# Attention with 64-query half tiles of 128 local keys, a column of ones in V, and the global queries as fifth steps of the same pipeline

## The chip, the core and the metric

The kernel runs on one core of a Trainium2 chip. The core has TensorE (PE, the matmul array, with a weight load that the profile lists as PEld), VectorE (DVE), ScalarE (ACT), GpSimd (POOL) and SyncE (SP, which here only issues DMAs). Each engine runs its own list of instructions in order; semaphores tie the lists together. The metric is the device time of one execution, in microseconds (us).

## The reference

Three layers follow each other: an attention of 512 local and 32 global positions (4 batches, 8 heads, head size 64), a routed expert layer, and a gated convolution layer. The change touches the attention alone:

```python
k_all = concat([k_g, k_l]); v_all = concat([v_g, v_l])
out_g = sm(scale * q_g @ k_all.T) @ v_all            # 32 global queries see all 544 keys
s_ll  = where(abs(i - j) <= 32, scale * q_l @ k_l.T, -1e9)
s_lg  = scale * q_l @ k_g.T                           # a local query sees 32 global keys
out_l = sm(concat([s_lg, s_ll])) @ concat([v_g, v_l]) # and local keys at most 32 away
x     = concat([out_g, out_l])                        # then expert layer, then convolution layer
# sm(s): s -= max(s); e = exp(s); e / (sum(e) + 1e-9)
```

All arithmetic here is float32.

## The kernel before

Heads are worked on in pairs: the 64 numbers of two heads lie on partitions 0 to 63 and 64 to 127. There are 16 pairs. Local queries stand in four tiles of 128 (`t`); such a tile sees 192 local keys (its own 128 and 32 on either side) and 32 global ones, 224 in all. `u` is the head within the pair.

For each pair PE does, in `period` (L717 to L724 in the listing): `scores` of the next pair (L688, eight calls of 224 columns, two heads in the two halves of the array's rows), `turn` of head 0 (probabilities transposed by an identity: L697 the first 128 keys, L699 the other 96, four calls each), `weigh` of the pair before's head 1 (L713 with the first 128 keys, L714 with the 96), `turn` of head 1, and `weigh` of head 0. In the profile a float32 matmul call is two MATMULs, and a transpose is one. The scores stand in PSUM banks 0 to 3, the transposed probabilities in banks 4 and 5 (one copy only), the results in banks 6 and 7.

DVE adds the mask and takes the negated maximum in one custom instruction for each 128x224 tile (`negated_max`, L1048), which also moves the scores to SBUF, copies bank 4 to `l_pta` (L1056), and divides a whole pair's result by the row sums (`normalize`, L1061, L1063, L1065). ACT takes the exponentials with their sums (L1395) and copies bank 5 to `l_ptb` (L1386). PE may turn the next head only when both copies are made.

After the 16 pairs the global queries follow as a phase of their own, in eight groups `k` of four heads (32 queries each, 128 rows): `g_scores` (L649, L650; 544 keys, the two pairs in the two halves of the array's columns), `g_turn` (L660, L661), `g_weigh` (L674, L676: four heads one behind the other, ten MATMULs each). Their probabilities are divided by DVE before they are turned (`g_probabilities`).

The order on each engine is the order in which the Python writes it; twelve of the sixteen periods stand in a loop. SP loads keys and queries into a ring of four pairs, and the values after; POOL issues the loads of the global phase's own keys and values (`g_k`, `g_v`), the stores of `x_rows`, and the load of `win`. Behind the attention PE transposes the rows of X for the router (`turn_tiles`, L761, then L775), and SP starts the loads of the experts' weights once the last `g_weigh` is done.

Of the kernel before, what the change touches and what calls it, by code (L numbers as in the profile page):

```python
# [37 lines left out]
WK = P + 2 * WINDOW  # L38
TK = SG + WK
VB = TK - P  # L40
# [14 lines left out]
COPY_AT = 2  # L55
PACE = 3
HIGHEST = 3.0e38
NRING = 4
PERIODS = NPAIR // NRING - 1
# [20 lines left out]
NC_CONST = C_MASK + NT * TK  # L80


def program(nc, qg, kT, v, ql, kw, va, vb, wg, w1, w2, w_in, w_out, cw, cst, out):
# [4 lines left out]
    with ctx:  # L88
# [37 lines left out]

        ends["local"] = ends["x"]

        l_q = [place("local", f"l_q{i}", [P, SL]) for i in range(NRING)]
        l_k = [place("local", f"l_k{i}", [P, NT, TK]) for i in range(NRING)]  # L130
        l_va = [place("local", f"l_va{i}", [P, NT, P]) for i in range(NRING)]
        l_vb = [place("local", f"l_vb{i}", [P, NT, P]) for i in range(NRING)]
        l_p = [[place("local", f"l_p{i}{u}", [P, NT, TK]) for u in range(2)] for i in range(2)]
        l_pta = [place("local", f"l_pta{u}", [P, NT, P]) for u in range(2)]
        l_ptb = [place("local", f"l_ptb{u}", [P, NT, P]) for u in range(2)]
        negmax = place("local", "negmax", [P, NRING, 2, NT])
        rowsum = place("local", "rowsum", [P, NRING, 2, NT])
        rowsum_e = place("local", "rowsum_e", [P, NRING, 2, NT])
        inv = place("local", "inv", [P, NRING, 2, NT])
        ends["globin"] = ends["const"]  # L140
        g_q = place("globin", "g_q", [P, NPAIR, 2 * SG])
        g_k = place("globin", "g_k", [P, NPAIR, S])
        g_v = place("globin", "g_v", [P, NPAIR, NT, P])
        g_vt = place("globin", "g_vt", [SG, NPAIR, P])
        zeros = place("globin", "zeros", [P, DM])
        ends["glob"] = ends["local"]
        g_p = [place("glob", f"g_p{i}", [P, S]) for i in range(2)]
        g_pt = place("glob", "g_pt", [P, NT + 1, P])
        g_max = place("glob", "g_max", [P, NG])
        g_negmax = place("glob", "g_negmax", [P, NG])  # L150
        g_sum = place("glob", "g_sum", [P, NG])
        g_sum_e = place("glob", "g_sum_e", [P, NG])
        g_inv = place("glob", "g_inv", [P, NG])
# [32 lines left out]
        assert ends["route"] <= ends["local"], (ends["route"], ends["local"])  # L186
# [17 lines left out]
        assert ends["globin"] <= ends["win"]  # L204
        win = place("win", "win", [P, DC, F2])
        ends["split"] = (nc.sbuf_usable_end - 2 * DC * F2 * 4) // 32 * 32
        assert ends["split"] >= ends["units"]
# [40 lines left out]
        gk_in = [sem(f"gk_in{k}") for k in range(NG)]  # L248
        gv_in = [sem(f"gv_in{k}") for k in range(NG)]
        lqk_in = [sem(f"lqk_in{i}") for i in range(NRING)]  # L250
        lv_in = [sem(f"lv_in{i}") for i in range(NRING)]
        s_ready = sem("s_ready")
        masked = sem("masked")
        max_ready = sem("max_ready")
        p_ready = sem("p_ready")
        gs_ready = sem("gs_ready")
        gmax_raw = sem("gmax_raw")
        gmax_ready = sem("gmax_ready")
        ge_done = sem("ge_done")
        gden = sem("gden")  # L260
        gp_ready = sem("gp_ready")
        gt_ready = sem("gt_ready")
        gta_copied = sem("gta_copied")
        gtb_copied = sem("gtb_copied")
        go_ready = sem("go_ready")
        t_ready = sem("t_ready")
        ta_copied = sem("ta_copied")
        tb_copied = sem("tb_copied")
        o_ready = sem("o_ready")
        den = sem("den")  # L270
        normed = sem("normed")
        xg_copied = sem("xg_copied")
# [77 lines left out]
        def of_pair(x, pair):  # L350
            return x[pair] if isinstance(pair, int) else x[bass.ds(pair, 1)].rearrange("a p s -> p (a s)")

        def load_keys(sp, pair, i):

            sp.dma_start(l_k[i][:].rearrange("p t k -> p (t k)"), of_pair(kw, pair)).then_inc(lqk_in[i], 16)

        def load_queries(sp, pair, i):
            sp.dma_start(l_q[i][:], of_pair(ql, pair)).then_inc(lqk_in[i], 16)

        def load_values(sp, pair, i):  # L360

            sp.dma_start(l_va[i][:].rearrange("p t k -> p (t k)"), of_pair(va, pair)).then_inc(lv_in[i], 16)
            sp.dma_start(l_vb[i][0:VB].rearrange("p t k -> p (t k)"), of_pair(vb, pair)).then_inc(lv_in[i], 16)

        def load_global_keys(eng, k):

            eng.dma_start(g_k[:, 2 * k:2 * k + 2], kT[2 * k:2 * k + 2].rearrange("a p s -> p a s")
                         ).then_inc(gk_in[k], 16)

        def load_global_values(eng, k):  # L370
            for a in range(2 * k, 2 * k + 2):
                eng.dma_start(g_v[:, a], v[a, 0:SL].rearrange("(c p) d -> p c d", p=P)).then_inc(gv_in[k], 16)
            eng.dma_start(g_vt[:, 2 * k:2 * k + 2], v[2 * k:2 * k + 2, SL:S].rearrange("a p d -> p a d")
                         ).then_inc(gv_in[k], 16)
# [47 lines left out]
        def _(sp):  # L422
            load_keys(sp, 0, 0)
            load_queries(sp, 0, 0)
            sp.dma_start(consts[:], cst).then_inc(const_in, 16)
            for pair in range(1, NRING):
                load_keys(sp, pair, pair)
                load_queries(sp, pair, pair)
                load_values(sp, pair - 1, pair - 1)
# [3 lines left out]
            def reload_keys(pair, i):  # L433

                sp.wait_ge(s_ready, pair + (1 - NRING + BIAS))
                load_keys(sp, pair, i)
                load_queries(sp, pair, i)

            def reload_values(pair, i):

                sp.wait_ge(o_ready, pair * 2 + (2 - 2 * NRING + BIAS))
                load_values(sp, pair, i)

            load_values(sp, NRING - 1, NRING - 1)
            reload_keys(NRING, 0)
            with sp.Fori(0, PERIODS - 1) as j:
                for i in range(NRING):
                    reload_keys(j * NRING + (NRING + 1 + i), (i + 1) % NRING)
                    reload_values(j * NRING + (NRING + i), i)
            for pair in range(NPAIR - NRING, NPAIR):  # L450
                if pair + 1 < NPAIR:
                    reload_keys(pair + 1, (pair + 1) % NRING)
                reload_values(pair, pair % NRING)
            sp.wait_ge(go_ready, NG)
# [36 lines left out]
        def _(pool):  # L491

            pool.wait_ge(pads_zero, 1)
# [3 lines left out]

            pool.wait_ge(pads_zero, 2)
            for u in range(2):
                r = slice(DH * u, DH * u + DH)  # L500
                pool.dma_start(g_q[r, :, SG * u:SG * u + SG], qg[:, r].rearrange("a p s -> p a s")).then_inc(gq_in, 16)
            def store_batch(b, pairs):
                pool.wait_ge(normed, pairs + BIAS)
# [3 lines left out]
            for k in range(NG):  # L507
                pool.wait_ge(o_ready, PACE * k + 2 + BIAS)
                load_global_keys(pool, k)
                load_global_values(pool, k)  # L510
                if k in (2, 5):
                    store_batch(k // 3, H // 2 * (k // 3 + 1))
            store_batch(2, 3 * H // 2)
            pool.wait_ge(normed, 3 * H // 2 + 2 + BIAS)
            pool.dma_start(win[:], w_in.rearrange("(c p) f -> p c f", p=P)).then_inc(win_in, 16)
            store_batch(3, NPAIR)
            pool.wait_ge(xg_copied, 1)
# [3 lines left out]
            pool.wait_ge(go_ready, NG)  # L521
# [103 lines left out]
        def _(pe):  # L625
            pe.sem_inc(s_ready, BIAS)
            pe.sem_inc(t_ready, BIAS)
            pe.sem_inc(o_ready, BIAS)
# [10 lines left out]
            def g_scores(k):  # L639
                i = k % 2  # L640
                pe.wait_ge(gk_in[k], 16)

                if k < 2:
                    pe.wait_ge(max_ready, HEADS + BIAS)
                else:
                    pe.wait_ge(ge_done, k - 1)
                for a in range(2):
                    o = slice(2 * SG * a, 2 * SG * a + 2 * SG)
                    mm(ps[o, 2 * i, :], g_q[:, 2 * k + a, :], g_k[:, 2 * k + a, 0:512], start=True, stop=True)  # L649
                    last = mm(ps[o, 2 * i + 1, 0:S - 512], g_q[:, 2 * k + a, :], g_k[:, 2 * k + a, 512:S],  # L650
                              start=True, stop=True)
                last.then_inc(gs_ready, 1)
# [10 lines left out]
            def g_weigh(k):  # L663
                b = k // 2
                if k == 0:
                    pe.wait_ge(normed, NPAIR - 1 + BIAS)
# [978 lines left out]
```

## Time and profile before

| | us |
|---|---|
| median of 3 runs | 728.49 (727.95 to 728.78) |
| the profiled execution | 729.33 |
| its span | 727.5 |
| PE busy | 670.9 (92%) |
| DVE busy | 522.7 (72%) |
| ACT busy | 366.4 (50%) |
| POOL busy | 224.1 (31%) |

The span runs from the first to the last instruction of that one execution. The chain of waits is followed back from the last instruction; a stretch that the chain gives to PE can't be shortened by any other engine. Clock 1.00 in a row means that TensorE ran at 2.4 GHz, 0.50 at 1.2 GHz.

### The profile page before, as it was taken

Reading aid. Unit: us, or ns where it says so; the run is one execution under the profiler, and the core shown is the slowest. Engines: PE = TensorE matmul, PEld = TensorE weight load, DVE = VectorE, ACT = ScalarE, POOL = GpSimd, SP = SyncE. Lnnn points to the kernel's source line nnn. Section 1 sums busy time; section 2 is a strip of 40 time slices with the busy share of each in tenths; the row PEclk is TensorE's granted clock in tenths of the full one; section 3 lists DMA queues with packets and bytes.
Section 4 is the critical chain, followed back from the end, with each engine's and each line's share of the span. In section 5 each row is a group of like instructions: output and inputs, shape, how many; then the busy total and the mean of one; then the engine's idle time right before and its main releaser. Section 6 shows DMA issues by size and latency. Waiting matters only on the chain.

```text
span 727.5 us, 12816 instructions
## 1 busy us (share of the span) xinstructions
PE 670.9 (92%) x3892; PEld 550.5 (76%) x3892; DVE 522.7 (72%) x970; ACT 366.4 (50%) x648; POOL 224.1 (31%) x189
## 2 busy tenths in 40 slices
PE   3999999899945999999999999997499999999997
PEld 2899999666434788888888888886278888888886
DVE  2667676443374989888998898894649878777672
ACT  2676776112103687777877787774242232222321
POOL 1132230002415455545554555442812011000000
PEclk9999999999965999999999999999689999999999
DMA  9989983202871010808621717400221021010102
GB/s 263 288 264 320 329 275 118 115 2 101 337 271 44 25 49 29 288 29 288 215 91 40 278 39 274 159 29 16 88 58 45 15 72 43 0 58 0 58 1 72
DMA packets 35965, 92.49 MB, mean 127 GB/s; under 512 B 3360, under 2 KB 3360, under 8 KB 35936
## 3 DMA queue, kind: packets, MB, share of 16 engines
q1 hardware_dynamic: 25024, 59.87, 24.1%
q0 software_dynamic: 7744, 26.48, 11.3%
q10 hardware_dynamic: 3168, 5.77, 2.1%
q8 instruction: 16, 0.26, 0.1%
q14 instruction: 13, 0.11, 0.0%
HBM read 76.90 MB, written 15.20 MB: 127 GB/s over the span
## 4 chain that ended last, share of the span: by engine, by line
PE 90%; DVE 4%; DMA 2%; issue 2%; POOL 1%; ACT 1%; SPq 0%; DVEq 0%; POOLq 0%; ACTq 0%
PE ps L854 20%; PE ps L856 20%; PE ps L855 20%; PE ps L714 4%; PE ps L688 4%; PE ps L713 4%; PE ps L885 3%; PE ps L674 3%; PE ps L697 2%; PE ps L775 2%; PE ps L699 2%; DMA l_q<-ql 2%; PE ps L863 1%; DVE y_g L1293 1%; PE ps L649 1%
## 5 line engine op out<-in xcount | busy, mean ns | idle before, releaser
L1444 ACT CAST w_h<-slots 128x1024 fp32r x88 | 92.0, 1049 | 47.6 <-PE ps L856 25.5
L1450 ACT CAST w_h<-slots 128x1024 fp32r x88 | 89.0, 1051 | 40.5 <-PE ps L856 27.4
L1249 DVE TENSOR_TENSOR w_l<-slots,w_h 128x1024 fp32r<-128x1024 f32 x66 | 87.6, 1375 | 12.0 <-ACT w_h L1444 8.8
L1256 DVE TENSOR_TENSOR w_l<-slots,w_h 128x1024 fp32r<-128x1024 f32 x66 | 77.8, 1230 | 16.5 <-ACT w_h L1450 16.0
L1524 ACT ACTIVATE h_buf<-ps 128x512 f32<-128x512 f32 x32 | 19.2, 601 | 123.2 <-PE ps L856 108.2
L551 POOL TENSOR_TENSOR w_l<-slots,w_h 128x1024 fp32r<-128x1024 f32 x22 | 54.6, 2483 | 73.6 <-ACT w_h L1444 73.6
L854 PE MATMUL ps<-w_h,b_hTh 128*128 128x512 f32 x176 | 71.7, 408 | 2.6 <-DVE b_hTl L1243 2.6
L854 PE MATMUL ps<-w_h,b_xTh 128*128 128x512 f32 x176 | 71.5, 406 | 1.8 <-DVE b_xTl L1236 1.6
L1048 DVE CUSTOM_DVE_ANT_0 l_p<-ps,consts 128x224 f32<-128x224 f32 x128 | 42.2, 386 | 42.9 <-PE ps L688 36.2
L558 POOL TENSOR_TENSOR w_l<-slots,w_h 128x1024 fp32r<-128x1024 f32 x22 | 57.9, 2632 | 43.0 <-ACT w_h L1450 43.0
L856 PE MATMUL ps<-w_h,b_xTl 128*128 128x512 f32 x176 | 69.9, 397 | 0.0
L855 PE MATMUL ps<-w_l,b_xTh 128*128 128x512 f32 x176 | 69.8, 396 | 0.0
L856 PE MATMUL ps<-w_h,b_hTl 128*128 128x512 f32 x176 | 69.4, 395 | 0.0
L855 PE MATMUL ps<-w_l,b_hTh 128*128 128x512 f32 x176 | 69.3, 394 | 0.0
L1395 ACT ACTIVATE l_p<-l_p,negmax 128x224 f32<-128x224 f32 x128 | 60.0, 471 | 9.7 <-DVE negmax L1048 9.3
L617 POOL COPY h_buf<-h_g 128x32 f32<-128x32 f32 x32 | 6.8, 214 | 147.3 <-DVE c_buf L1340 147.1
L854 PE MATMUL ps<-yT_h,win_h 128*128 (+1 forms) x128 | 50.6, 395 | 0.5 <-DVE yT_l L1297 0.5
L854 PE MATMUL ps<-wout_h,gl_h 128*128 128x512 f32 x128 | 51.0, 399 | 0.0
L856 PE MATMUL ps<-yT_h,win_l 128*128 (+1 forms) x128 | 50.6, 396 | 0.0
L855 PE MATMUL ps<-yT_l,win_h 128*128 (+1 forms) x128 | 50.5, 395 | 0.0
L856 PE MATMUL ps<-wout_h,gl_l 128*128 128x512 f32 x128 | 50.1, 392 | 0.0
L855 PE MATMUL ps<-wout_l,gl_h 128*128 128x512 f32 x128 | 49.9, 390 | 0.0
(225 smaller groups left out, 1503.8 us busy)
## 6 DMA issues: line engine op xcount, KB each, us to landing
slots<-w SPq DMA_DIRECT2D x16, 2048.0 KB, 11.0
l_k<-kw SPq DMA_DIRECT2D x16, 448.0 KB, 7.1
y_sorted<-b_y ACTq DMA_DIRECT2D x22, 256.0 KB, 2.9
g_k<-kT POOLq DMA_DIRECT2D x8, 544.0 KB, 5.4
l_q<-ql SPq DMA_DIRECT2D x16, 256.0 KB, 8.3
l_va<-va SPq DMA_DIRECT2D x16, 256.0 KB, 3.2
g_v<-v POOLq DMA_DIRECT2D x16, 256.0 KB, 6.6
x_rows<-X POOLq DMA_DIRECT2D x4, 1024.0 KB, 7.4
```

The source lines that it names most:

```text
L551: nc.gpsimd.tensor_tensor(w_l[:, u, :], unit_of(at, False, u), w_h[:, u, :].bitcast(F32), ALU.subtract).then_inc(w_lo_pool, 1)
L558: nc.gpsimd.tensor_tensor(w_l[:, u, :], unit_of(at, True, u), w_h[:, u, :].bitcast(F32), ALU.subtract).then_inc(w_lo_pool, 1)
L688: last = mm(ps[:, 2 * u + t // 2, at:at + TK], l_q[i][r, P * t:P * t + P], l_k[i][r, t, :], start=True, stop=True)
L854: mm(o, a_h, b_h, start=start, stop=False)
L855: mm(o, a_h, b_l, start=False, stop=False)
L856: return mm(o, a_l, b_h, start=False, stop=stop)
L1048: last = vec.tensor_tensor_reduce(out=l_p[i % 2][u][:, t, :], in0=ps[:, 2 * u + t // 2, t % 2 * TK:t % 2 * TK + TK], in1=consts[:, C_MASK ...
L1249: vec.tensor_tensor(w_l[:, u, :], unit_of(at, False, u), w_h[:, u, :].bitcast(F32), ALU.subtract).then_inc(w_lo_dve, 1)
L1256: vec.tensor_tensor(w_l[:, u, :], unit_of(at, True, u), w_h[:, u, :].bitcast(F32), ALU.subtract).then_inc(w_lo_dve, 1)
L1395: last = sca.activation(at, at, ACT.Exp, bias=negmax[:, i, u, t:t + 1], scale=-1.0, accum_out=rowsum[:, i, u, t:t + 1])
L1444: sca.copy(w_h[:, u, :], unit_of(at, False, u)).then_inc(w_hi, 1)
L1450: sca.copy(w_h[:, u, :], unit_of(at, True, u)).then_inc(w_hi, 1)
```

## The change

A tile of 128 queries is split into two halves of 64. Each half sees 128 local keys (its own 64 and 32 on either side), so that the tile is 160 columns wide (128 local, 32 global) rather than 224. The two halves go to the two halves of the array's columns, the two heads to the two halves of its rows. V gets a 65th column of ones, so that the sum of a row's exponentials comes out of the same matmul, and the divisions come after it. The values of the global keys lie in `l_vg` as a block matrix (128x260, one block for each tile), so that one call covers four tiles. Two pairs and their four heads' global queries make a group of five steps, which run in one pipeline; `g_scores` reads the keys that the local scores read. The rings get six pairs; there is no loop. PSUM banks 6 and 7 now hold one head each in turn.

```diff
-            def scores(pair, i, loads):
+            def scores(pair):
...
+                pe.wait_ge(qk_in[i], 32 * (pair // NRING + 1))
+                if pair >= 1:
+                    pe.wait_ge(max_ready, sub(pair - 1, 1) + 1)
+                    if pair % 2 == 0:
+                        pe.wait_ge(p_ready, sub_g(pair // 2 - 1) + 1)
                 for t in range(NT):
                     at = t % 2 * TK
...
+                    for u, r in enumerate(rows):
+                        mm(ps[0:HQ, 2 * u + t // 2, at:at + TK], l_q[i][r, q[0]], k[r], start=True, stop=True)
+                        mm(ps[HQ:P, 2 * u + t // 2, at:at + WK], l_q[i][r, q[1]], beside[r], start=True, stop=True)
+                    for u, r in enumerate(rows):
+                        last = mm(ps[HQ:P, 2 * u + t // 2, at + WK:at + TK], l_q[i][r, q[1]], k[r, WK:TK],
                                   start=True, stop=True)
...
+            def g_scores(g):
...
+                for a in range(2):
+                    pair = 2 * g + a
+                    k, q = l_k[pair % NRING], g_q[:, pair, :]
+                    o = slice(2 * SG * a, 2 * SG * a + 2 * SG)
+                    mm(ps[o, 0, SG:P], q, k[:, SG:P], start=True, stop=True)
+                    mm(ps[o, 0, P:SL], q, k[:, TK:NT * TK].rearrange("p (t k) -> p t k", k=TK)[:, :, 0:P],
+                       start=True, stop=True)
+                    last = mm(ps[o, 1, 0:2 * SG], q, k[:, NT * TK - SG:NT * TK + SG], start=True, stop=True)
...
+            def turn(pair, u):
...
                 for t in range(NT):
-                    last = nc.tensor.transpose(ps[0:VB, 5, P * t:P * t + P], l_p[i % 2][u][:, t, P:TK], ident)
+                    last = mm(ps[SG * t:SG * t + SG, 5, 0:P], p[:, TK * t + WK:TK * t + TK], ident,
+                              start=True, stop=True)
...
-                    mm(o, l_pta[u][:, t, :], l_va[i][:, t, d], start=True, stop=False)
-                    last = mm(o, l_ptb[u][0:VB, t, :], l_vb[i][0:VB, t, d], start=False, stop=True)
+                mm(ps[:, bank, 0:NT * VW], l_ptb[turned][:], l_vg[i][:, u].rearrange("p t d -> p (t d)"),
+                   start=True, stop=False)
+                for t in range(NT):
+                    for h in range(2):
+                        last = mm(ps[HQ * h:HQ * h + HQ, bank, VW * t:VW * t + VW],
+                                  l_pta[turned][:, t, HQ * h:HQ * h + HQ], l_va[i][:, 2 * t + h, u, :],
+                                  start=False, stop=t == NT - 1)
...
+            for g in range(NG):
+                for a in range(2):
+                    if a == 0:
+                        scores(2 * g + 1)
+                    else:
+                        g_scores(g)
+                    turn(2 * g + a, 0)
+                    if a == 1:
+                        weigh(2 * g, 1)
+                    elif g >= 1:
+                        g_weigh(g - 1)
+                    turn(2 * g + a, 1)
+                    weigh(2 * g + a, 0)
+                if g + 1 < NG:
+                    scores(2 * g + 2)
+                g_turn(g)
+                weigh(2 * g + 1, 1)
```

`g_weigh` now writes its four heads to the four quarters of the array's columns (four chunks of 128 keys, L703, and a last one of 64, L706). SP has eight DMAs for each pair rather than four: keys 352 KB, queries 256 KB, local values 520 KB, four small ones for `l_vg` (16 KB each) and one for `l_vt`. A group takes PE two `scores`, one `g_scores`, four `turn`, one `g_turn`, four `weigh` and one `g_weigh`.

PE, one pair inside the loop of the kernel before (the scores of the next pair stand at L688):

```order
52 L688 MATMUL ps<-l_k_72,l_q_68 128x224 [waits max_ready]
53 L688 MATMUL ps<-l_k_72,l_q_68 128x224 x7
54 L693 REGISTER_ALU
55 L697 MATMUL ps<-consts,l_p_81 128x128 [waits tb_copied,ta_copied,p_ready]
56 L697 MATMUL ps<-consts,l_p_81 128x128 x3
57 L699 MATMUL ps<-consts,l_p_81 96x128 x4
58 L713 MATMUL ps<-l_va_74,l_pta_86 128x64 [waits tb_copied,ta_copied]
```

PE of the kernel after, at the border of two groups (the last tile of `scores` of pair 2, `g_turn`, `weigh`, and the first tile of `scores` of pair 3):

```order
84 L629 MATMUL ps<-l_k_73,l_q_67 64x32 x2
85 L669 MATMUL ps<-consts,g_p 128x128 [waits ta_act,tb_copied,p_ready]
86 L669 MATMUL ps<-consts,g_p 128x128 x3
87 L670 MATMUL ps<-consts,g_p 64x128
88 L685 MATMUL ps<-l_vg_84,l_ptb_104 128x260 [waits normed,ta_act,tb_copied]
89 L689 MATMUL ps<-l_va_78,l_pta_102 64x65 x8
90 L626 MATMUL ps<-l_k_74,l_q_68 64x160 [waits max_ready,qk_in3]
91 L627 MATMUL ps<-l_k_74,l_q_68 64x128
```

Before, a turn and a weighing stand between two `scores` on all sides; now the `scores` of pair 3 come straight behind the weighing of pair 1's head 1, and wait for `max_ready`, the maxima of pair 2's head 1.

DVE of the kernel before, where the last maxima of a pair's head 1 are taken (L1048) and the pair before it is divided (L1061 to L1065):

```order
60 L1048 ISA l_p_82,negmax<-ps,consts 128x224
61 L1048 ISA negmax 128x1
62 L1059 ISA
63 L1061 TENSOR_SCALAR rowsum_e<-rowsum 128x8 [waits p_ready,o_ready]
64 L1062 REGISTER_ALU
65 L1063 RECIPROCAL inv<-rowsum_e 128x8 [waits den]
66 L1065 ISA [waits den]
67 L1065 TENSOR_TENSOR X<-ps,inv 128x2x4x64
68 L1055 REGISTER_ALU
69 L1056 COPY l_pta_86<-ps 128x512 [waits t_ready]
```

DVE of the kernel after, at the same border (L1028 copies the group's turned probabilities, L1035 to L1040 divide pair 1's head 1, L1012 takes the maxima of pair 2's head 1):

```order
110 L1028 COPY l_pta_102<-ps 128x512 [waits o_ready,t_ready]
111 L1035 TENSOR_SCALAR den<-ps 128x4 [waits o_ready]
112 L1037 RECIPROCAL inv<-den 128x4 [waits den_ready]
113 L1040 TENSOR_TENSOR X<-ps,inv 128x4x64 [waits inv_ready]
114 L1012 ISA l_p_98,negmax<-ps,consts 128x160 [waits t_ready,s_ready]
115 L1012 ISA negmax 128x1
116 L1012 ISA l_p_98,negmax<-ps,consts 128x160
```

Before, the maxima came ahead of the division; here the division of a head whose weighing PE has just issued stands ahead of the maxima.

## Rows read from the trace of the kernel before

**Rows 1.** The page's part 4: shares of the chain by engine

```profile
PE 90%; DVE 4%; DMA 2%; issue 2%; POOL 1%; ACT 1%; SPq 0%; DVEq 0%; POOLq 0%; ACTq 0%
```

**Rows 2.** Busy time by engine (PE, PEld, DVE, ACT, POOL), clock, DMA share, GB/s

```profile
50.00:75.00 25.00, 25.00 (x229) 23.71 (x226) 16.48 (x69) 18.25 (x67) 8.92 (x13) 1.00 0.96 306
```

**Rows 3.** The chain of waits over one period: start, us, what

```profile
59.28 1.71 PE ps L688 x16
60.99 0.59 PE ps L697 x4
61.58 0.44 PE ps L699 x4
...
63.75 0.45 PE ps L697 x4
...
66.36 1.71 PE ps L688 x16
```

**Rows 4.** The same chain at the start, in the global phase and behind the attention

```profile
2.66 12.65 DMA l_q<-ql
15.40 3.37 PE ps L688 x16
...
23.82 1.71 PE ps L688 x16
...
151.72 1.01 PE ps L649 x4
...
155.98 0.59 PE ps L660 x4
...
175.33 3.65 PE ps L761 x32
178.97 3.53 PE ps L775 x8
...
213.41 0.26 PE ps L833 x8
...
220.11 0.88 PE ps L848 x17
```

**Rows 5.** PE in time, at a change of shape: start, us, engine, line, tile, count

```profile
148.37 0.29 PE L676 MATMUL ps<-g_vt,g_pt 32*32 32x64 f32 x2
148.59 0.24 PE L674 MATMUL ps<-g_v,g_pt 128*32 128x64 f32 x1
```

**Rows 6.** DVE and PE in time, the last pair's division

```profile
132.60 0.17 DVE L1061 TENSOR_SCALAR rowsum_e<-rowsum 128x8 f32<-128x8 f32 x1 [1.00 <-PE ps L714]
132.81 0.20 DVE L1063 RECIPROCAL inv<-rowsum_e 128x8 f32<-128x8 f32 x1
133.04 0.69 DVE L1065 TENSOR_TENSOR X<-ps,inv 128x512 f32<-128x512 f32 x1
133.65 0.14 DVE L1030 TENSOR_SCALAR g_sum_e<-g_sum 128x1 f32<-128x1 f32 x1
...
134.59 0.44 PE L660 MATMUL ps<-consts,g_p 128*128 128x128 f32 x2 [2.02 <-DVE g_p L1034]
```

**Rows 7.** DVE in time, two masked maxima one behind the other

```profile
61.30 0.39 DVE L1048 CUSTOM_DVE_ANT_0 l_p<-ps,consts 128x224 f32<-128x224 f32 x1 [2.15 <-PE ps L688]
...
61.61 0.39 DVE L1048 CUSTOM_DVE_ANT_0 l_p<-ps,consts 128x224 f32<-128x224 f32 x1
```

**Rows 8.** From a turn by way of the copy to the weighing

```profile
166.31 0.27 PE L661 MATMUL ps<-consts,g_p 128*32 128x128 f32 x1
166.62 0.69 DVE L1039 COPY g_pt<-ps 128x512 f32<-128x512 f32 x1 [2.64 <-PE ps L661]
...
167.41 0.27 PE L674 MATMUL ps<-g_v,g_pt 128*32 128x64 f32 x2 [0.83 <-DVE g_pt L1039]
```

**Rows 9.** Columns as in rows 2, behind the idle stretch of rows 6

```profile
135.60:139.00 3.40, 3.40 (x24) 2.09 (x21) 2.08 (x6) 0.84 (x3) 0.00 (x0) 0.50 0.77 290
139.00:142.00 3.00, 3.00 (x34) 2.19 (x34) 0.14 (x1) 0.14 (x1) 0.00 (x0) 1.00 0.00 0
```

More of the change, by code:

```diff
@@ L135, in program @@
[L135 to L153, printed above, removed]
+        ends["ring"] = ends["const"]
@@ new lines, in program @@
+        ends["local"] = ends["x"]
+        l_p = [[place("local", f"l_p{i}{u}", [P, NT * TK]) for u in range(2)] for i in range(2)]
+        l_pta = [place("local", f"l_pta{i}", [P, NT, P]) for i in range(2)]
+        l_ptb = [place("local", f"l_ptb{i}", [P, P]) for i in range(2)]
+        g_p = place("local", "g_p", [P, GK])
+        negmax = place("local", "negmax", [P, 2, 2, NT])
+        den = place("local", "den", [P, 2, NT])
+        inv = place("local", "inv", [P, 2, NT])
+        g_max = place("local", "g_max", [P, NG])
@@ L155, in program @@
+        g_negmax = place("local", "g_negmax", [P, NG])
+        g_den = place("local", "g_den", [P, NG])
+        g_inv = place("local", "g_inv", [P, NG])
         ends["route"] = ends["x"]
@@ L348, in program @@
         storedg = sem("storedg")
[L350 to L374, printed above, removed]
+        def sub(pair, u):
+            return 5 * (pair // 2) + 2 * (pair % 2) + u
@@ L634, in _ @@
             mm = nc.tensor.matmul
[L639 to L652, printed above, removed]
@@ L715, in weigh @@
                 last.then_inc(o_ready, 1)
-            def period(p, i, loads, first=False, more=True):
-                if more:
-                    scores(p + 1, (i + 1) % NRING, loads + (1 if i + 1 == NRING else 0))
-                turn(p * 2, i, 0)
-                if not first:
-                    weigh(p + -1, (i - 1) % NRING, 1, loads - (1 if i == 0 else 0))
-                turn(p * 2 + 1, i, 1)
-                weigh(p, i, 0, loads)
-            scores(0, 0, 1)
-            pe.wait_ge(const_in, 16)
@@ L728, in _, with g_weigh @@
-            period(0, 0, 1, first=True)
-            with pe.Fori(0, PERIODS) as j:
-                for i in range(1, NRING + 1):
-                    period(j * NRING + i, i % NRING, j + (1 if i < NRING else 2))
-            for p in range(NPAIR - NRING + 1, NPAIR):
-                if p + 1 == NPAIR:
-                    pe.wait_ge(gq_in, 32)
-                    g_scores(0)
-                period(p, p % NRING, NPAIR // NRING, more=p + 1 < NPAIR)
-            for k in range(NG):
-                if k + 1 < NG:
-                    g_scores(k + 1)
-                if k == 0:
-                    weigh(NPAIR - 1, (NPAIR - 1) % NRING, 1, NPAIR // NRING)
-                else:
-                    g_weigh(k - 1)
-                g_turn(k)
+            def g_weigh(g):
+                n = sub_g(g)
+                ready_to_weigh(n)
+                bank, turned = 6 + n % 2, n % 2
+                for c in range(NT + 1):
+                    for h in range(H // 2):
+                        i, u = (2 * g + h // 2) % NRING, h % 2
+                        o = ps[SG * h:SG * h + SG, bank, 0:VW]
+                        if c < NT:
+                            mm(o, l_pta[turned][:, c, SG * h:SG * h + SG], l_va[i][:, 2 * c, u, :],
+                               start=(c == 0), stop=False)
+                        else:
+                            last = mm(o, l_ptb[turned][0:2 * SG, SG * h:SG * h + SG], l_vt[i][:, u, :],
+                                      start=False, stop=True)
+                last.then_inc(o_ready, 1)
@@ new lines, in g_normalize @@
+            def g_normalize(g):
+                n, b = sub_g(g), g // 2
+                act.wait_ge(ginv_ready, g + 1)
+                for h in range(H // 2):
+                    r, at = slice(SG * h, SG * h + SG), DH * (H // 2 * (g % 2) + h)
+                    last = sca.activation(X[SG * b:SG * b + SG, GT, at:at + DH], ps[r, 6 + n % 2, 0:DH], ACT.Copy,
+                                          scale=g_inv[r, g:g + 1])
+                last.then_inc(g_normed, 1)
+            for u in range(2):
+                exponentials(0, u)
@@ new lines, in _ @@
+            for g in range(NG):
+                for a in range(2):
+                    pair = 2 * g + a
+                    copy_turned(sub(pair, 0), P, False)
+                    if a == 0:
+                        exponentials(pair + 1, 0)
+                        if g >= 1:
+                            g_normalize(g - 1)
+                    else:
+                        g_exponentials(g)
+                    copy_turned(sub(pair, 1), P, True)
+                    if a == 0:
+                        exponentials(pair + 1, 1)
+                copy_turned(sub_g(g), 2 * SG, False)
+                if g + 1 < NG:
+                    for u in range(2):
+                        exponentials(2 * g + 2, u)
@@ new lines @@
+    values = np.ones((NPAIR, P, NX, 2, VW), np.float32)
+    for x in range(NX):
+        values[:, :, x, :, 0:DH] = padded_values[:, HQ * x:HQ * x + WK]
+    tails = np.ones((NPAIR, 2 * SG, 2, VW), np.float32)
+    tails[:, 0:SG, :, 0:DH] = global_values
+    tails[:, SG:, :, 0:DH] = local_values[:, SL - SG:]
+    global_queries = np.zeros((P, NPAIR, 2, SG), np.float32)
+    for u in range(2):
+        global_queries[DH * u:DH * u + DH, :, u] = turned(inputs["q_g"])[:, DH * u:DH * u + DH].transpose(1, 0, 2)
```

479 lines of the change are left out of this document (218 added, 261 removed).

## The prediction

> **What bounds the kernel now.** I read the chain's shares first: PE has 90% of them [rows 1]. The busy time by engine of a stretch of the local attention comes second: PE is busy for all 25.00 us, DVE for 16.5, ACT for 18.3, the 16 DMA engines for 0.96 of it [rows 2]. So PE alone sets the pace here, though the loads have little room. Third comes the chain inside one period [rows 3]: 7.08 us for a pair (66.36 - 59.28), made of scores 1.71, a first turn 0.59 + 0.44, two weighings of 1.73 (the last L699 ends at 62.02, the next L697 starts at 63.75) and a second turn of about 0.9. The global phase has a period of its own: from g_scores at 151.72 to g_turn at 155.98 [rows 4] are 4.26 us, less 1.10 for g_scores leaves 3.16 for one g_weigh; with a g_turn of 0.70 a group is 4.96 us. The whole attention runs until 175.33, where L761 begins. What lies behind it starts from semaphores that end the attention and is the same code, so that I move it as a block.
>
> **PE's prices.** A float32 matmul of 512 columns costs 3.53 / 8 = 0.441 us for each L775 [rows 4], that is 0.86 ns a column. By it the 16 matmuls of scores (224 columns, 0.193 each) would be 3.09 us one by one; they take 1.71, so the two row halves run side by side. The four L649 would be 1.76 and take 1.01: so do the two column halves. The eight L833, in four column quarters, take 0.26 us together [rows 4], 0.033 each. Rows and columns divided at once, in four quarters, no row shows. A change of shape costs: two L676 of 64 columns (0.055 each by the rate) fill 0.22 us (148.37 to 148.59) [rows 5], so about 0.10 for each change; the first turn behind scores agrees (0.59 against 0.45) [rows 3]. The Trainium skill (TensorEngine Tiling (Array Packing), Key Properties) says that a change of the tiling mode drains TensorE; it gives no time, and the trace agrees with it at those 0.10 us.
>
> **Part by part on PE.** Each call is two matmuls.
> - scores: each quarter of the array gets 320 columns a tile (2 x 160, or 2 x 128 + 2 x 32), 0.275 us, and the short ones may wait for their weights; I take 0.30. Four tiles 1.20, a weight load 0.05, a change 0.10: **1.35** against 1.71.
> - turn: four transposes 0.45 + 0.05; L662 is eight matmuls of 128 columns in four column quarters, 2 x 0.11; two changes: **0.93**, as before.
> - weigh: L685 0.11 for weights and 2 x 0.224 for 260 columns, L689 sixteen of 65 columns (0.056) in two column halves, 0.45 + 0.05, two changes: **1.25** against 1.73.
> - g_scores: 2 x 544 columns, 0.94 + 0.15: 1.08, as before. g_turn 0.70, as before.
> - g_weigh: ten matmuls of 0.057 in each quarter, three changes and weights: **0.82** against 3.16.
>
> Whole: from scores of pair 1 on, 15 x 1.35 + 8 x 1.08 + 32 x 0.93 + 8 x 0.70 + 32 x 1.25 + 8 x 0.82 = 110.8 us. Before, the same stretch is 159.9 us (175.33 - 15.40).
>
> **The wait that it adds.** At each of the seven borders of groups, PE's scores of the odd pair wait for the maxima of the even pair's head 1. DVE has the division of the weighing just issued ahead of them. So from the end of weigh: 0.2 until DVE sees it (L661, 0.11 us of columns from 166.31, answered at 166.62 [rows 8]); division 0.21 + 0.23 [rows 6] + 0.34 for 256 of 512 elements (512 are followed after 0.61; an element is (0.69 - 0.39) / 288 = 1.04 ns by [rows 6, 7]); four maxima of 160 elements at 0.245 each (0.31 at 224 [rows 7], less 64 x 1.04 ns) = 0.98, and 0.12 to be read out. PE's own drain covers 0.1. That is 0.2 + 0.78 + 1.1 - 0.1 = **2.0 us idle, 7 times, 14.0**. Behind it are queued the turns of the next group. The copy is a smaller one: L661's start to L674's is 1.10 us [rows 8]; between the end of a turn and the next one stands now a weigh of 1.25, which covers it, or a g_weigh of 0.82, which lacks 0.17: 7 x 0.17 = 1.2. DVE's load of a group is 16 maxima x 0.245, three copies x 0.61, four divisions x 0.78, g's maximum and inverse 1.2: 10.1 of some 16 us, so not the bound. ACT's exponentials get shorter and lose their sum.
>
> **The clock.** PE was idle 2.02 us at 132.6 to 134.59 [rows 6], and then stood at 0.50 for 3.4 us [rows 9]; half of that, 1.7 us, is lost. The seven new gaps are as long. Nothing else in the attention has one so long, so I can't tell how often; I take 4 of 7: **6.8 us** (0 to 11.9). At the start the first period costs 8.42 (15.40 to 23.82) where 7.08 less one weighing is 5.35 [rows 3, 4], since its scores take 3.37 at the low clock: 3.0 us, kept.
>
> **Issue.** A group has 273 matmuls (2 x 48, 4 x 12, 4 x 18, 12 + 5 + 40) in some 16 us; two pairs and a global group before had 181 (2 x 64 + 53) in 19.1. They come in bursts (48 in scores, 40 in g_weigh). Nearest row: seventeen L848 in 0.88, 0.05 each [rows 4]; the eight L833 say 0.033. At 0.05, scores behind the gap (nothing queued) would be 2.4 rather than 1.35, and g_weigh 2.0 rather than 0.82; with a little from L689 that is 2.5 a group, 20 in all. Being nearer to L833 in kind, I take 0.4 at each border, **2.8** (0 to 20).
>
> The Trainium skill (TensorE: Matmul & The Clock Gate, Wait — 56ns, not 53.3ns?) puts the least distance of two matmuls at about 25 ns. By this scores would stay at 48 x 25 = 1.2 us and g_weigh come to 1.0, some 1.5 us over all; no row here shows so dense a run, and my 2.8 does without it.
>
> **Loads.** A pair needs 352 + 256 + 520 + 64 + 33 = 1225 KB; before it was 448 + 256 + 256 + 192 and 544 for the global copy, 1696 KB in 7.08 us at 0.96 of the DMA engines [rows 2]. At 16 us for two pairs they are hidden, as are SP's eight issues; the ring refills a group after it is done with, two groups ahead. Exposed is the start: PE waits for the second pair's queries, 12.65 us from issue [rows 4], with 2240 KB up to them. Now 2458 KB stand there (the constants shrink from 832 to 624 KB, but the first pair's values have been moved ahead): x 1.10, **+1.3, with five more issues 1.5** (0 to 4).
>
> **Sum.** 15.40 + 1.5 + 110.8 + 14.0 + 1.2 + 3.0 + 6.8 + 2.8 + 0.3 (the last division ahead of L761; g's scaling lies beside L761) = 155.8, where 175.33 stood: -19.5 of a profiled execution of 729.33. The median stands 0.84 below that execution; 728.5 - 19.5 = **709**.
>
> **Rivals.**
> - The gaps don't bring the clock down and nothing is short of instructions: 709 - 6.8 - 2.8 = 699.5, down to 697 if the quarters take 0.275. For it: one gap and one fall [rows 6, 9] are no rule. 22%.
> - Issue bounds the bursts: the full 20 us in place of 2.8, 726; half of it 717. For it: L848. Against: L833, and the queue fills while a turn or L685 runs. 18%, 716 to 728.
> - Slower: quarters don't run side by side. If no more than two matmuls run at once in scores, each is 0.60 a tile: 15 x 1.2 = +18. If column halves also wait for each other's weights (the 128 weight columns of L713 and L714 make 16 matmuls of 64 columns 1.73, 0.108 each where the columns alone are 0.055 [rows 3]), L689 costs 0.9: 32 x 0.45 = +14. Both: 709 + 32 = 741. It decides from +19.5 on. Against: L649 and L833. 12%.
> - The first loads or the ring come late, or the maxima wait is doubled (a second wait in each group): 8 x 2 = 16, 725. Against: the order of DVE, with g's maximum between g_scores and a turn. 3%.
> - The forecast, 45%: 702 to 717.
>
> **Range and chances.** 80%: 696 to 730, which leaves out most of the slower case and the lowest end. A change under 0.2% (1.5 us) can't be told from none. Faster 0.86, same 0.02 (issue and clock together at their ends), slower 0.12.
>
> **What would show it.** L761 begins near 156. The first L626 of a border stands idle about 2.0 us, released by DVE's negmax L1012, seven times. L626 to L629 take 1.2 to 1.3 us for 48 matmuls at full clock: at 2.4 the quarters fail. L703 and L706 end within 0.8 us. L689's sixteen take 0.5; 0.9 says that weights bound them. The clock in windows behind the gaps tells whether 4 of 7 is right. If PE is idle ahead of L659 as well, DVE or ACT are slower than their rows. I am wrong if the period of a group is over 19.5 us or under 15.

## The result and the profile after

The changed kernel takes **704.9 us** (median of 4 runs, 702.89 to 705.67) where the kernel before takes 728.22 in runs of the same chip: a ratio of 0.967 [0.964, 0.970], 23.3 us less. The forecast was 709, with 696 to 730 around it.

The page's part 1 and the shares of the chain, after (before: [rows 1]):

```profile
PE 636.3 (90%) x4628; PEld 506.1 (72%) x4628; DVE 509.0 (72%) x993; ACT 354.9 (50%) x560; POOL 205.1 (29%) x161
...
PE 87%; DVE 6%; issue 2%; DMA 1%; POOL 1%; SPq 1%; ACT 1%; POOLq 0%; DVEq 0%; ACTq 0%
```

DVE has gone from 4% of the chain to 6%, PE from 90% to 87%. Where DVE comes in, the list of PE's waits says (total us, times, longest):

```profile
PE ps L626 <- DVE negmax L1012: 14.0, 7, 2.0
PE ps L626 <- DMA l_q<-ql: 10.5, 2, 5.8
```

The chain from one border of groups to the next shows it from inside (start, us, what):

```profile
30.50 0.64 PE ps L689 x16
31.17 0.17 DVE den L1035
31.36 0.19 DVE inv L1037
31.61 0.31 issue
31.92 0.24 DVE l_p L1012
...
32.73 0.24 DVE l_p L1012
32.99 0.14 issue
33.12 0.32 PE ps L626
```

PE ends a weighing at 31.14 and starts the scores of the odd pair at 33.12. Between them stand the division (its last step, the product L1040, runs in the "issue" of 0.31, since no semaphore of this chain names it) and four masked maxima. Along the same chain, the even pair's weighing of head 1 returns at

```profile
37.50 0.64 PE ps L685 x2
...
53.89 0.64 PE ps L685 x2
...
71.77 0.64 PE ps L685 x2
```

so a group, two pairs and a global group in one, takes 16.39 us, or 17.88 when PE's clock has fallen in it. Before, two pairs were 2 x 7.08 and a global group 4.96: 19.12 [rows 3, 4].

PE in time inside that group, to be read against [rows 3, 5]:

```profile
34.59 0.66 PE L659 MATMUL ps<-consts,l_p 128*128 128x128 f32 x4
35.19 0.43 PE L662 MATMUL ps<-consts,l_p 128*32 128x128 f32 x8
35.43 0.64 PE L703 MATMUL ps<-l_va,l_pta 128*32 128x65 f32 x32
36.00 0.32 PE L706 MATMUL ps<-l_vt,l_ptb 64*32 64x65 f32 x8
36.52 0.63 PE L659 MATMUL ps<-consts,l_p 128*128 128x128 f32 x4 [0.21 <-DVE l_pta L1028]
...
37.43 0.71 PE L685 MATMUL ps<-l_vg,l_ptb 128*128 128x260 f32 x2
38.07 0.69 PE L689 MATMUL ps<-l_va,l_pta 128*64 128x65 f32 x16
38.58 0.33 PE L642 MATMUL ps<-l_k,g_q 128*64 128x96 f32 x2
```

Starts tell more than durations here, which overlap. The 48 matmuls of scores fill 33.12 to 34.59, 1.47 us: the quarters do run side by side. A turn and the weighing behind it, from 36.52 to 38.58, are 2.06. The g_weigh that took 3.16 us [rows 4] is over in 0.9 (35.43 to 36.31, then 0.21 of waiting for the copy).

The clock, in two of three such stretches that begin shortly behind a gap (columns as in rows 2; compare [rows 9]; the third is 101.4 to 104.8):

```profile
67.30:70.70 3.40, 3.32 (x71) 2.63 (x64) 1.77 (x10) 0.76 (x3) 0.00 (x0) 0.63 0.00 0
135.50:138.90 3.40, 3.40 (x78) 2.91 (x72) 1.39 (x9) 0.58 (x3) 0.00 (x0) 0.62 0.03 5
```

Three of the seven borders (the third, the fifth and the seventh) brought the clock down to 0.50 inside these stretches, which is 1.2 GHz; at the other four, with gaps just as long, it stood at 1.00. A fall costs 17.88 - 16.39 = 1.49 us.

The start and the end of the attention:

```profile
3.44 1.23 SPq L356
...
4.71 1.27 SPq L356
...
7.97 5.24 DMA l_q<-ql
...
13.30 0.49 PE ps L626 x2
...
150.22 0.30 ACT X L1369
...
151.51 0.70 DVE r_xT L1091
...
152.26 1.97 PE ps L745 x16
154.22 3.53 PE ps L759 x8
```

Scores of pair 1 begin at 13.30 (before: 15.40 [rows 4]). The first turn of X's tiles stands in the timeline of PE at

```profile
149.95 1.94 PE L745 MATMUL ps<-consts,X 128*128 128x128 f32 x16 [0.19 <-DVE X L1040]
```

25.4 us ahead of its counterpart L761 at 175.33 [rows 4]. The profiled executions differ by 24.4 (729.33 and 704.95): 1 us is given back behind the attention. 0.6 of it shows here, L759 starting 4.27 us behind L745 where L775 started 3.64 behind L761, because ACT first scales the last global group (L1369, four times 0.3 us, which the kernel before didn't have) and only then copies the turned tiles. The rest can't be told from chance: in the six traces of the kernels that are alike from there on, this one among them, the time from the first L745 to the end was 551.1 to 553.4 us.

### The profile page after: what moved, and what is told of

Its sections match the earlier page's. It is cut to its first block, busy times and chain, and to the rows that moved or that the text cites. A ratio compares the mean times of both kernels' runs of the same rounds, so it can differ in the third digit from the quotient of the medians.

```text
span 703.2 us, 14036 instructions
## 1 busy us (share of the span) xinstructions
PE 636.3 (90%) x4628; PEld 506.1 (72%) x4628; DVE 509.0 (72%) x993; ACT 354.9 (50%) x560; POOL 205.1 (29%) x161
## 4 chain that ended last, share of the span: by engine, by line
PE 87%; DVE 6%; issue 2%; DMA 1%; POOL 1%; SPq 1%; ACT 1%; POOLq 0%; DVEq 0%; ACTq 0%
PE ps L838 21%; PE ps L839 21%; PE ps L840 21%; PE ps L689 3%; PE ps L869 3%; PE ps L685 3%; PE ps L659 3%; PE ps L626 2%; PE ps L759 2%; PE ps L662 2%; PE ps L847 1%; DVE l_p L1012 1%; DVE y_g L1261 1%; PE ps L922 1%; PE ps L627 1%
## 5 line engine op out<-in xcount | busy, mean ns | idle before, releaser
L1415 ACT CAST w_h<-slots 128x1024 fp32r x88 | 92.0, 1049 | 47.4 <-PE ps L840 25.4
L526 POOL TENSOR_TENSOR w_l<-slots,w_h 128x1024 fp32r<-128x1024 f32 x22 | 54.3, 2469 | 74.9 <-ACT w_h L1415 74.9
L533 POOL TENSOR_TENSOR w_l<-slots,w_h 128x1024 fp32r<-128x1024 f32 x22 | 56.6, 2571 | 39.5 <-ACT w_h L1421 39.5
L1012 DVE CUSTOM_DVE_ANT_0 l_p<-ps,consts 128x160 f32<-128x160 f32 x128 | 33.7, 321 | 31.2 <-PE ps L629 24.5
L1345 ACT ACTIVATE l_p<-l_p,negmax 128x160 f32<-128x160 f32 x128 | 44.2, 417 | 16.3 <-DVE negmax L1012 15.2
```

The lines of the kernel that those rows point to most:

```text
L526: nc.gpsimd.tensor_tensor(w_l[:, u, :], unit_of(at, False, u), w_h[:, u, :].bitcast(F32), ALU.subtract).then_inc(w_lo_pool, 1)
L533: nc.gpsimd.tensor_tensor(w_l[:, u, :], unit_of(at, True, u), w_h[:, u, :].bitcast(F32), ALU.subtract).then_inc(w_lo_pool, 1)
L1012: last = vec.tensor_tensor_reduce(out=p[:, TK * t:TK * t + TK], in0=ps[:, 2 * u + t // 2, t % 2 * TK:t % 2 * TK + TK], in1=consts[:, mask: ...
L1345: last = sca.activation(at, at, ACT.Exp, bias=negmax[:, pair % 2, u, t:t + 1], scale=-1.0)
L1415: sca.copy(w_h[:, u, :], unit_of(at, False, u)).then_inc(w_hi, 1)
```

## The experiments

All were timed against the kernel before in runs of the same chip (median 728.2 to 728.5 there).

**The maxima ahead of the division and the copy.** In DVE's code:

```diff
                 if g + 1 < NG:
                     negated_max(2 * g + 2, 0)
-                copy_turned(sub_g(g))
-                normalize(2 * g + 1, 1)
-                if g + 1 < NG:
                     negated_max(2 * g + 2, 1)
+                copy_turned(sub_g(g))
+                normalize(2 * g + 1, 1)
```

> Theory (the border gap is DVE's order: the division of the weighing just issued stands ahead of the maxima): with the maxima of pair 2g+2's head 1 taken right behind those of head 0, ahead of the copy and the division, the seven gaps of 2.0 us fall to about 0.3 each, -12 us, and with no long gap the clock stays at 1.00 through the attention, where it fell three times: another -4.5. In all -14 to -17, near 689. Rival (another wait stands right behind, such as the exponentials of that head or the copy of the group's probabilities, now later): the gap only moves to the first turn or to g_weigh, and the time falls by less than 5 us.

Measured: 687.8 us, ratio 0.943 [0.938, 0.948], 17.1 below the changed kernel. Its waits, and the clock over the whole of the attention:

```profile
PE ps L626 <- DVE negmax L1012: 3.3, 7, 0.5
...
30.00:135.00 105.00, 100.20 (x1927) 75.94 (x1921) 72.32 (x360) 66.25 (x197) 3.05 (x4) 1.00 0.58 184
```

The gap is 0.5 us rather than 2.0, and the clock never falls. The group is 14.87 us. The first L745 comes 14.3 us earlier:

```profile
135.60 1.94 PE L745 MATMUL ps<-consts,X 128*128 128x128 f32 x16 [0.19 <-DVE X L1040]
```

Seven groups that are 1.52 shorter make 10.6 us, three falls 4.5: 15.1, of which this execution lost 0.9 again at its start, where the queries came 0.5 later and PE's low speed lasted longer (the turn behind the first g_scores began at 24.37 rather than 23.51). So the gaps and the falls came from a place in DVE's order, not from the work. The profiled executions differ by 15.4, the medians by 17.1; what goes beyond the attention I didn't trace.

**Only the division moved behind the maxima**, the copy left ahead of them:

```diff
                 copy_turned(sub_g(g))
-                normalize(2 * g + 1, 1)
                 if g + 1 < NG:
                     negated_max(2 * g + 2, 1)
+                normalize(2 * g + 1, 1)
```

> The changed kernel with the maxima of an even pair's head 1 ahead of the division alone; the copy of the turned block stays ahead of them. Theory: the gap at each border loses the division, 0.78 us of 2.0, so 1.2 remains: 7 x 0.78 = 5.5 less; if gaps of 1.2 us no longer bring the clock down, 3 x 1.5 = 4.5 more. 704.9 - 5.5 = 699.4, or 694.9. Rival: the falls of the clock have nothing to do with the gaps' length, but with the gaps being there at all: three or four falls stay, and 699 to 701.

Measured: 691.3 us, ratio 0.948 [0.943, 0.953]; 694.9 was expected for the branch that held. In the trace the attention ends 11.0 us earlier (the first L745 at 138.97), near the 10.0 of that branch.

```profile
PE ps L626 <- DVE negmax L1012: 7.5, 7, 1.1
```

The gap shrank to 1.1 (by 0.93 rather than 0.78, since the division's hand-over goes too), the group to 15.46, and no stretch of the attention was below clock 1.00. The rival, that the falls belong to the gaps whatever their length, is out for gaps of 1.1 us. The times of the other executions agree with the profiled ones: the granted clock over the whole execution was 0.961 to 0.965 in all four of this kernel and of the one above, 0.955 in all four of the changed kernel.

**A longer gap**: two copies of 512 columns, one behind the other, ahead of the maxima at each border. The copies overwrite `zeros`, so DVE's first maximum also waits, at the start, until the DMA that reads it is done (`last_zeroed`).

```diff
             dve.wait_ge(const_in, 16)
+            dve.wait_ge(last_zeroed, 16)
...
                 if g + 1 < NG:
+                    for i in range(2):
+                        vec.tensor_copy(zeros[:], consts[:, 0:DM]).then_inc(pads_zero, 1)
+                        dve.wait_ge(pads_zero, 2 * g + i + 3)
                     negated_max(2 * g + 2, 1)
```

> Two copies of 128x512 within SBUF, one waiting for the other, stand on DVE between the division and the maxima at each of the seven borders (0.4 to 0.7 us each with the wait). Theory: the path runs through here, so the gap grows by all of it, 0.8 to 1.4 us to about 3.1, +6 to +10 us; the gaps are then long enough that the clock falls behind more of the seven than the three before, up to +6 more. In all +6 to +16. Rival (the gap is set by something else that ends only a little earlier): under +3.

Measured: 711.5 us, ratio 0.976 [0.971, 0.981], 6.6 above the changed kernel, at the lower end.

```profile
PE ps L626 <- DVE negmax L1012: 26.3, 8, 5.8
...
67.50:72.60 5.10, 5.10 (x100) 3.99 (x93) 2.96 (x18) 3.02 (x11) 0.00 (x0) 0.67 0.08 11
```

One wait of 5.8 is at the start, where the added wait of DVE holds PE up; the seven at the borders are 20.5, 2.93 each. Groups without a fall take 17.31 (16.39 + 0.93), and four of seven have one (one of the four stretches is shown), at 1.2 to 1.6 us. The first L745 comes at 155.70, 5.75 later: 7 x 0.93 = 6.5 and about 1.1 for the falls, less 1.8 at the start, where PE's low speed ended sooner. With the runs above: gaps of 0.5 and 1.1 us brought no fall in 7 and 7, of 2.0 three in 7, of 2.9 four in 7. So the length matters between 1.1 and 2.0; that a longer gap brings more falls than one of 2.0, three against four don't show.

**The second pair's keys and queries first** (SP's order; the first pair's values behind them).

```diff
+            load_keys(sp, 1)
 ...
-                load_keys(sp, pair)
+                if pair > 1:
+                    load_keys(sp, pair)
```

> SP issues the keys and queries of pair 1 before the values of pair 0, which took it from 2.27 to 7.30 us. Theory (the start is now bound by SP's issues, five of which are small and slow): these queries are issued near 3 us rather than 7.97 and land near 9 to 10 rather than 13.2, so PE's second scores start 3 us earlier and the time falls by 2 to 4 us. Rival (the start is bound by the bytes, or the low clock that ends near 22.9 takes it back): less than 1 us.

Measured: 703.2 us (701.4 to 705.2), ratio 0.964 [0.959, 0.969]. That is 1.7 below the changed kernel, between the theory's 2 to 4 and the rival's less than 1, and inside the spread of the runs. In the trace nothing is kept: the first turn of X starts at 149.97, as in the changed kernel (149.95). The queries land at 10.46 (2.67 + 7.79) rather than 13.21, and the first global scores start at 19.56 rather than 22.20, 2.6 earlier. But they still run at half speed (until the turn at 21.90, 2.3 us rather than 1.25), and so does a part of the turn behind them (its L659 take 0.81 rather than 0.59), which together takes back 1.3; that is the rival's low clock. The other 1.5 go because the clock then fell at four borders, the first of them here, where the changed kernel had three:

```profile
31.80:36.90 5.10, 5.10 (x104) 4.45 (x104) 2.03 (x11) 2.59 (x9) 0.00 (x0) 0.67 0.48 156
```

**Both edits together** (the maxima ahead of the copy and the division, the second pair's keys and queries first), to see whether the 2.6 us are real once no fall can take them back:

> The changed kernel with the maxima ahead of the division and the copy (as the run at 687.8) and with the second pair's keys and queries issued ahead of the first pair's values. Theory: in the profile of the keys-first kernel the first global scores begin 2.6 us earlier (19.56 against 22.20 us), and one more fall of the clock (four for three) took 1.5 back. Without the gaps there is no fall to take anything, so the whole of it is kept: 687.8 - 2.6 = 685.2, 684 to 686.5. Rival: what starts earlier waits later for the first pair's values or in the ring, and nothing is kept: 687 to 689.

Measured: **685.5 us** (684.5 to 686.8), ratio 0.941 [0.936, 0.946]. By the medians 2.3 are kept, by the traces 3.5 (the first turn of X starts at 132.14 rather than 135.60, groups 14.87 in both), of which 0.9 is the slower start of the execution it is compared with. The theory holds; this kernel is the fastest of the study, 19.4 us below the changed one.

**The kernel before with its other loads held back** until the second pair's queries are in.

```diff
+                if pair == 1:
+                    sp.wait_ge(lqk_in[1], 32)
```

> The kernel before, with SP waiting for pair 1's keys and queries before it issues anything more. Theory (these queries took 12.65 us because the loads queued right behind them shared the engines, not because of the bytes ahead): they land near 11 rather than 15.3, and the time falls by 2 to 4 us. Rival (my prediction's rule: only the 2240 KB ahead of them count): they still land near 15, and nothing is gained, or a little lost since the next loads are late.

Measured: 727.6 us (725.7 to 733.2), ratio 0.999 [0.996, 1.003]: no difference that can be told. Its chain says what the time could not:

```profile
2.66 11.14 DMA l_q<-ql
13.90 3.37 PE ps L690 x16
...
173.82 3.65 PE ps L763 x32
```

The queries land in 11.14 us rather than 12.65 [rows 4], and the turn of X starts 1.5 us earlier (173.82 against 175.33). That looks like the theory, but it isn't shown. The kernel of the next experiment issues the same loads at the start as the kernel before and holds none back, and in its trace the same queries land as early:

```profile
2.66 11.19 DMA l_q<-ql
```

So 12.65 and 11.19 are two executions of the same loads, and the 1.5 us can be chance. Neither the theory nor the rival is decided.

**The kernel before with g_weigh alone in column quarters.** Each head writes its own quarter of PE's columns, and sixteen small copies put the result into X.

```diff
-                for h in range(4):
-                    a, u, at = h // 2, h % 2, DH * (4 * (k % 2) + h)
-                    for c in range(NT):
-                        mm(ps[o, 6, at:at + DH], g_pt[:, c, SG * h:SG * h + SG], ...
+                for c in range(NT + 1):
+                    for h in range(4):
+                        a, u, o = h // 2, h % 2, ps[SG * h:SG * h + SG, 6, DH * k:DH * k + DH]
+                        if c < NT:
+                            mm(o, g_pt[:, c, SG * h:SG * h + SG], ...
```

> The kernel before with one thing changed: g_weigh writes its four heads to the four column quarters of PE, and sixteen small copies bring the result into X. Theory: a g_weigh falls from 3.16 to about 0.9, and a global group from 4.96 us to the next bound, DVE's and ACT's loop of maximum 0.87, exponentials 0.98, sum, inverse and scaling 0.85, some 3.0 with the hand-overs: 8 x 1.96 = 15.7 less; the small copies add 16 x 0.2 - 0.6 = 2.6. 728.5 - 13 = 715.5, 713 to 719. Rival: without the merging the global part keeps most of its time, since its loop through DVE and ACT is what bounds it (4 us a group or more): 721 to 729.

Measured: 714.0 us (712.7 to 719.6), ratio 0.979 [0.974, 0.984]. The chain in the global phase:

```profile
148.56 1.02 PE ps L649 x4
...
149.66 0.58 PE ps L673 x32
150.25 0.24 PE ps L676 x8
...
151.19 1.02 PE ps L649 x4
```

A group takes 2.63 us (151.19 - 148.56) where it took 4.96: PE's own work, the loop through DVE and ACT bounds nothing, and the bound of 3.0 that I had expected isn't there. (Only in the last two groups does PE wait for DVE's copy, 0.8 us each, as in the kernel before.) The g_weigh is 0.82 (0.58 + 0.24). Against 8 x 2.33 = 18.6 saved stand the small copies, which hold up the turn of X by more than their 2.6 told: sixteen of them, on the chain from

```profile
161.06 0.28 DVE X L1044
```

to 165.85, 0.28 us each. With them the first L775 starts about 9.2 us behind the first L761 rather than 3.64 [rows 4], which is 5.6 lost. The rival (the merging is needed for it) falls: 14.2 of the 23.3 us are had without any merging.

The profiled execution, 719.64, is the slowest of the five and 5.6 above their median. Its chain shows where: PE stood at half speed until about 30 us, while the clock read 1.00, where it stood so until about 21 in the profiled execution of the kernel before.

```profile
28.57 1.04 PE ps L697 x4
...
36.47 0.59 PE ps L697 x4
```

From the scores of the second pair to those of the fourth it takes 20.8 us (13.95 to 34.76), where the kernel before took 15.5 (15.40 to 30.93) with the same code.

**The local attention alone**: the changed kernel without its global steps. The global queries' result is left out; tile 16 of X, which it fills, gets a copy of tile 0.

```diff
+            for p in range(NPAIR):
+                if p + 1 < NPAIR:
+                    scores(p + 1)
+                turn(p, 0)
+                if p >= 1:
+                    weigh(p - 1, 1)
+                turn(p, 1)
+                weigh(p, 0)
+            weigh(NPAIR - 1, 1)
```

> The changed kernel without the global attention's steps (tile 16 of X gets a copy of tile 0 instead), so that the local attention stands alone. Theory: PE bounds it, and a pair takes 1.47 + 2 x 0.94 + 2 x 1.25 = 5.85 us, where the kernel before takes 7.08; no gap of PE at a border, since the maxima stand well ahead, and no fall of the clock: the last turn ends near 112 us, and the whole takes 664 to 669. Rival: at 1225 KB for each pair the loads bound a pair (in the kernel before 1696 KB took 7.08 us at 0.96 of the DMA engines, 240 KB for each us; 5.85 us needs 210): PE waits for l_k, l_q or l_va, and a pair takes 6.3 or more, the whole 672 or more.

Measured: 664.4 us (663.0 to 667.8). One pair in the chain, and ten in the table of busy times:

```profile
39.55 0.59 PE ps L649 x4
...
45.41 0.59 PE ps L649 x4
```

```profile
38.00:97.00 59.00, 59.00 (x1100) 43.12 (x1099) 41.96 (x232) 37.25 (x112) 3.05 (x4) 1.00 0.84 271
```

A pair takes 5.86 us (45.41 - 39.55) against 5.85 told and 7.08 before [rows 3]. PE doesn't stop once in 59 us, at a DMA share of 0.84: the loads don't bound it.

## Why the prediction was right

The forecast's mechanism (PE bounds; its blocks shrink; a wait for the maxima opens at each border and brings the clock down at some) held, and so did its largest terms. Several sizes were off and partly cancelled, so that the time came nearer than the terms were. It put the end of the attention at 155.8; it came at 149.95.

- **Blocks of PE (110.8 told).** Without the gap of 2.0 and the 0.21 of waiting for the copy a group is 14.18; 2 x 5.86 + 2.63 = 14.35 from the last two experiments is near it; told were 14.0. Scores took 1.47 rather than 1.35 and g_scores 1.25 rather than 1.08; why, no run shows. Turn, weigh, g_turn and g_weigh were within 0.1. Over eight groups 1.2 too little.
- **The gaps (14.0 told).** 14.0, seven times, 2.0 the longest; the place of the maxima behind the copy and the division is the cause, as the runs with them moved show (0.5, and 1.1 with the division alone behind them).
- **The copy (1.2 told).** Right in kind and size. The list of waits has L659 behind DVE's copy; [0.21] in the timeline above, about 1.4 in seven.
- **The clock (6.8 told, four of seven).** Three of seven at 1.49: 4.5. How many of seven I could only guess, and near it was luck. The link to the gap's length, on which I had one case, is now shown: none in 14 gaps of up to 1.1 us, 7 in 14 of 2.0, 4 in 7 of 2.9. Which of the gaps brings a fall stays open.
- **The low speed at the start (3.0 told).** 4.5. The first group, from 13.30 to 33.12, takes 17.8 without its gap, where the same blocks without a g_weigh would be 13.3. How long the low speed lasts differs from one execution to the next (see the run with g_weigh alone).
- **Issue (2.8 told, 0 to 20).** The step that failed in kind. Scores behind a gap, where nothing is queued, take the same 1.47 as elsewhere, and L703's 32 records stand within 0.57 us (35.43 to 36.00), 18 ns each. Seventeen L848 in 0.88 [rows 4] were the wrong row to fear. That the blocks are dearer by 1.2 and the start by 1.5 made up for it by chance. The Trainium skill (TensorE: Matmul & The Clock Gate, Wait — 56ns, not 53.3ns?) has about 25 ns as the least distance of two matmuls; in these column quarters the records stand closer, and the measurement decides.
- **The start (16.9 told).** The step that was off the most: 13.30. I scaled 12.65 us by the bytes ahead. But the queries are issued only at 7.97, behind the first pair's values (L356: 0.72, 1.23 and 1.27 us, and 0.62), and then land in 5.24. The rule itself fails: 2458 KB landed at 13.21 here, 2240 KB at 15.31 in the kernel before, and at 13.85 in the other trace of the same loads. So up to 1.5 of the 3.6 us can be that the one trace I started from was a late one; what sets the landing stays open.
- **Behind the attention (0 told).** 1.0 us given back, of which 0.6 is shown: the scaling of the last global group does stand in front of ACT's copies, not beside L761.

The sum of these against the 155.8: start -3.6, blocks +1.2, low speed at the start +1.5, issue -2.8, clock -2.3, copy +0.2, last division -0.1, which is -5.9 where -5.85 was measured; 1.0 comes back behind. The rivals: the gaps did bring the clock down, so 699.5 was not it; issue bound nothing; quarters run side by side, in scores and in L689 (sixteen in 0.51, 38.07 to 38.58).

**What each part of the change is worth**, from the pieces: half tiles and the column of ones (not separated here) take a pair from 7.08 to 5.86, 16 x 1.22 = 19.5 us. Column quarters take a global group from 4.96 to 2.63, 8 x 2.33 = 18.6. The start gives 2.1 between these two traces, 0.7 against the other trace of the same loads. Putting the global groups between the pairs saves PE almost nothing: a merged group without its waits is 14.18 where its parts are 14.35, and the gaps, the copy's wait and the falls cost 14.0 + 1.4 + 4.5. The kernel before had one gap and one fall of its own, 2.0 + 1.7 [rows 6, 9]. That makes 24.0 (19.5 + 18.6 + 2.1 - 19.9 + 3.7) of the 25.4 by which the attention ends earlier. The rest is about what the kernel before waits for DVE's copy in its last two global groups, 1.7 us, where the changed kernel has no such wait; the merged groups' 8 x 0.17 = 1.4 and the start's 1.5 more of low speed cancel. The merging pays in loads (the global attention reads the same K and V), which don't bound here. A kernel with half tiles and quarters but the two phases apart was not built; my estimate, from 109.20, where the local attention alone starts turning X, eight groups of 2.63, and the gap and fall of 3.7 where the phases meet, is 130 to 134, near the 132 of the fastest kernel.

## What to carry to other kernels

Two streams merged into one pipeline were worth the sum of their parts here only when, at every seam, the other engine's work that the next step waits for stood ahead of the work that nobody waited for yet: moving four maxima ahead of a division and a copy, no work saved, took off another 17.1 us, where the whole change took 23.3. A gap of 2 us costs its own length and, in 7 of 14 cases here, 1.5 us more of clock behind it; gaps of 1.1 us cost only themselves. Before pricing a load by the bytes ahead of it, see when its issue leaves the queue, and take its landing from more than one trace: the same loads took 12.65 and 11.19 us. The same holds for a gain of 1 to 2 us read from one pair of traces.

## What the runs showed of the hardware

- Four row-and-column quarters (64*64) run at once: 48 matmuls of 160, 128 and 32 columns in 1.47 us. The first four start within 0.02 us.
- At the start PE works at half speed while the granted clock reads 1.00: the chain of the changed kernel has four transposes of a turn at

```profile
16.09 1.04 PE ps L659 x4
...
23.51 0.59 PE ps L659 x4
```

  With the loads held back the granted clock did read 0.50 from 12 to 16 us:

```profile
12.00:16.00 4.00, 2.10 (x12) 2.10 (x14) 0.84 (x6) 3.17 (x14) 0.00 (x0) 0.50 0.36 95
```

  and the sixteen L690 took 3.37 us, no more than the L688 of [rows 4] at a reading of 1.00. The column doesn't tell everything about the speed of PE near the start, and the length of that low speed isn't fixed: it lasted until about 21 us in the trace of the kernel before and until about 30, with the same code up to there, in the one with g_weigh alone changed, which cost it 5.3 us.
- A DVE copy of 32 x 128 elements from PSUM costs 0.28 us: sixteen of them took 4.8 us.
